# Start of an attention and two-MLP kernel on TensorE: a group of scores placed earlier, two loads issued later, and seven identity products in the gaps

## The reference, cut to what matters

```python
for c in range(nc):                       # chunks of 32 queries
    k_full = np.concatenate([mem_k, k_ctx], axis=2)       # 8 + 16 + 32 + 8 keys
    scores = scale * np.matmul(q_c, k_full.transpose(0, 1, 3, 2))
    a = np.exp(scores - max); a = a / (np.sum(a) + 1e-09)
    out[:, :, c_start:c_end] = np.matmul(a, v_full)
...
h = np.maximum(np.maximum(x @ w1, x @ w2), x @ w3)        # 3072 x 512 x 768, three times
x2 = h @ w_out                                            # 3072 x 768 x 512
h = x2 @ w_in                                             # 3072 x 512 x 2048
g = np.where(h >= 1, h, np.where(h <= -1, 0.0, (h + 1) ** 2 / 4))
return g @ w_out2                                         # 3072 x 2048 x 512
```

## Time and profile before

| what | us |
|---|---|
| median of 3 runs | 960.1 |
| lowest and highest run | 959.87, 960.55 |
| the execution that was profiled | 960.76 |
| its span, first to last instruction | 959.0 |
| TensorE busy in the span | 944.0 |
| GpSimd, DVE, ACT busy | 455.7, 484.2, 434.9 |

### The profile page before, as it was taken

The page is one execution under the profiler, slowest core; times in us unless marked ns, Lnnn a source line. Parts: engine busy times, 40 slices in busy tenths (PEclk is TensorE's granted clock), DMA queues, the critical chain, the costliest instruction groups (busy, mean ns, idle before and its releaser), DMA issues.

```text
span 959.0 us, 19061 instructions
## 1 busy us (share of the span) xinstructions
PE 944.0 (98%) x7806; PEld 877.6 (92%) x7806; DVE 484.2 (50%) x755; ACT 434.9 (45%) x713; POOL 455.7 (48%) x628
## 2 busy tenths in 40 slices
PE   5999999999999999999999999999999999999998
PEld 5999999999999999999989899898999898989897
DVE  4673566667766695761344432545334453423232
ACT  3342343443433443432545555645556463645354
POOL 1668997868986593130232423333332323232321
PEclk9999999999999999999999999999999999999999
DMA  9777899999699778882536445445464443555321
GB/s 373 260 265 245 319 325 387 403 413 397 227 393 383 269 263 304 278 308 103 185 119 226 154 176 187 176 153 184 155 233 144 153 162 137 199 178 182 121 99 66
DMA packets 50327, 223.01 MB, mean 233 GB/s; under 512 B 5952, under 2 KB 10048, under 8 KB 42688
## 3 DMA queue, kind: packets, MB, share of 16 engines
q0 software_dynamic: 31936, 165.17, 48.1%
q1 hardware_dynamic: 18304, 56.63, 16.2%
HBM read 178.00 MB, written 43.78 MB: 231 GB/s over the span
## 4 chain that ended last, share of the span: by engine, by line
PE 95%; DMA 2%; POOL 2%; issue 1%; DVE 0%; ACT 0%; SPq 0%; POOLq 0%
PE mlp_ps L647 21%; PE mlp_ps L648 21%; PE mlp_ps L649 21%; PE attn_ps L649 4%; PE attn_ps L648 4%; PE attn_ps L647 3%; PE scores_ps L649 3%; PE scores_ps L648 3%; PE scores_ps L647 3%; PE attn_ps L640 3%; PE trans_ps L649 2%; PE trans_ps L648 2%; PE trans_ps L647 2%; PE scores_ps L611 2%; DMA wb<-wb_scratch 1%; PE trans_ps L620 1%
## 5 line engine op out<-in xcount | busy, mean ns | idle before, releaser
L936 ACT ACTIVATE up_m<-mlp_ps 128x384 f32<-128x384 f32 x292 | 142.3, 489 | 303.4 <-PE mlp_ps L649 275.0
L647 PE MATMUL mlp_ps<-yc,wa 128*128 128x384 f32 x472 | 160.2, 339 | 0.2 <-issue 0.2
L648 PE MATMUL mlp_ps<-yc,wa 128*128 128x384 f32 x472 | 158.5, 336 | 0.0
L649 PE MATMUL mlp_ps<-yc,wa 128*128 128x384 f32 x472 | 158.0, 335 | 0.0
L544 POOL CAST wo<-wo_raw 128x1024 fp32r<-128x1024 f32 x32 | 33.3, 1039 | 193.5 <-PE trans_ps L649 187.3
L523 POOL DMA_DIRECT2D wa<-wa_scratch x59 | 31.7, 538 | 192.5 <-PE mlp_ps L649 192.4
L647 PE MATMUL mlp_ps<-yc,wb 128*128 128x384 f32 x354 | 119.3, 337 | 0.4 <-DMA wb<-wb_scratch 0.4
L648 PE MATMUL mlp_ps<-yc,wb 128*128 128x384 f32 x354 | 118.9, 336 | 0.0
L649 PE MATMUL mlp_ps<-yc,wb 128*128 128x384 f32 x354 | 118.4, 334 | 0.0
L1537 DVE SCALAR_TENSOR_TENSOR ramp<-ramp,up_m 128x768 f32<-128x768 f32 x62 | 59.5, 959 | 109.1 <-ACT ramp L1187 109.1
L647 PEld LDWEIGHTS mlp_ps<-yc,wa 128*128 128x128 f32 x472 | 88.6, 188 | 7.0 <-ACT up_m L936 0.7
(11 more groups left out here) (178 smaller groups left out, 2178.7 us busy)
## 6 DMA issues: line engine op xcount, KB each, us to landing
wa<-wa_scratch POOLq DMA_DIRECT2D x59, 1024.0 KB, 5.3
wb<-wb_scratch POOLq DMA_DIRECT2D x59, 768.0 KB, 6.8
qk_raw<-qk_l SPq DMA_DIRECT2D x24, 768.0 KB, 8.5
wo_raw<-w_out POOLq DMA_DIRECT2D x32, 512.0 KB, 4.0
wa_scratch<-stage_a POOLq DMA_DIRECT2D x30, 512.0 KB, 5.0
v_raw<-v_l SPq DMA_DIRECT2D x24, 512.0 KB, 7.5
wb_scratch<-stage_a POOLq DMA_DIRECT2D x30, 384.0 KB, 6.9
y_raw<-y_scratch SPq DMA_DIRECT2D x8, 768.0 KB, 5.0
```

Source lines behind the costliest of these rows:

```text
L647: pe.matmul(out_ap, a_hi, b_hi, start=first, stop=False, skip_group_check=beside)
L648: pe.matmul(out_ap, a_lo, b_hi, start=False, stop=False, skip_group_check=beside)
L649: return pe.matmul(out_ap, a_hi, b_lo, start=False, stop=last, skip_group_check=beside)
L936: return act.activation(o, i, ACT.Copy)
```

## The change

There are three edits. First, on TensorE `scores` of group 3 goes from behind the first large product to ahead of it. Second, on SyncE the loads of weight piece 2 and of v of group 3 trade places, and a wait on `attn_done` 2 is put ahead of both. Third, a helper `keep_busy` issues products of the identity with itself (float32, 128x128) into PSUM that nothing reads before it is overwritten: one each behind the scores of groups 0 and 1, two behind those of group 2, one behind the first transposes (with a wait on `sub_done` 2, for the bank), and two behind the transposes of group 1.

```diff
@@ SyncE @@
             load_qk(3)
+            sp.wait_ge(attn_done, 2)
+            load_wa(2)
             load_v(3)
-            load_wa(2)
             load_wa(3)
@@ TensorE, first_tile @@
                     if f == 0:
                         scores_ready(n0, 0, 1)
+                        scores(n0, 0)
                     if r == 0 and j:
                         weighted_v(n0 + j - 1, j - 1)
                         scores(n0 + j, j)
                     layer1(0, 0, f, 0)
-                    if f == 0:
-                        scores(n0, 0)
@@ TensorE, prologue @@
+            def keep_busy(count, bank):
+
+                for _ in range(count):
+                    pe.matmul(bank[:, 0:P], ident[:, :], ident[:, :], start=True, stop=True)
+
             scores_ready(0, 0, 0)
             scores(0, 0)
+            keep_busy(1, trans_ps)
             scores_ready(1, 1, 0)
             scores(1, 1)
+            keep_busy(1, trans_ps)
             scores_ready(2, 2, 0)
             scores(2, 2)
+            keep_busy(2, trans_ps)
             transposes(0, 0)
+            pe.wait_ge(sub_done, 2)
+            keep_busy(1, mlp[0])
             weights_ready(0, 0, 0)
             pe.wait_ge(sub_done, GPT)
             weighted_v(0, 0)
             transposes(1, 1)
+            keep_busy(2, mlp[0])
             transposes(2, 0)
```

## The result

The changed kernel takes 978.1 us (median of six runs, 971.4 to 983.8), the kernel before 960.3 in the same comparison (six runs, 959.9 to 961.7). The ratio on record is 1.0174, with a 95% interval of 1.0152 to 1.0196: 1.7% slower (the quotient of the two medians is 1.0185). The execution that was profiled took 983.76 us with a span of 982.0 us; against the profiled execution of before it lost 23.0 us. It is the slowest of the six, so the trace shows more loss than the 17.8 us between the medians. The forecast was 959.1 us.

A forecast was written before the change was run, and what follows sets the result against it. TensorE was taken as the bound, so time won in the first 28 us passes to the end. The profiled 960.76 us less 1.66 us, the clock gain net of 0.68 us delay, gave 959.1 us; range 956.0 to 960.6.

The forecast's parts named there:

- The scores ahead of the large product: Scores of group 3, moved into TensorE's 0.90 us wait for `x_hi`, run from 21.15 to 22.26 us and cost nothing.
- The loads: SyncE's loads held back by 4.5 us, v of group 3 among them, were needed late; costed at nothing.
- Rival 3: Held loads make GpSimd late, so `wa` lands beyond its 4.7 us of slack; 962.8 us, slower; chance 0.06.
- The clock term: TensorE's clock rises at 25.7 us, with 8 of the first 14 large matmuls slow; net gain 1.66 us.
- The identity products: Seven float32 products in TensorE's prologue, 0.39 us each; those in waits cost nothing, two between transposes cost 0.68 us.
- The 0.68 us of delay at the transposes: Two products between transposes of groups 1 and 2 find no gap and move all behind by 0.68 us (0.42 to 0.94).
- Rival 1: Identity products raise TensorE's clock already in the prologue, so small products run faster; 955.3 to 957.9 us; chance 0.32.
- They cost nothing, even at 0.52: Products behind scores of groups 0 to 2 and the first transposes fit TensorE's waits of 0.6 to 1.4 us.

The follow-up runs named there:

- The first experiment: Kernel before plus seven tiny 32x1 identity products (28 TensorE instructions) ahead of the first scores; 974.7 us, ratio 1.013.
- the run with the whole shift: Changed kernel plus 57 tiny 32x1 identity products ahead of the first scores, shifting the stream by 256 instructions in all; 960.4 us, ratio to before 0.9996.

## Why the prediction was wrong, by its own steps

- **The scores ahead of the large product: right.** In the run with the scores alone they start at 21.27 us and the large product follows at 22.38, with no wait for `x_hi`; forecast were 21.15 and 22.43.
- **The loads: right.** They cost nothing, alone or with the scores. Rival 3 did not happen: `wa` has no wait of its own in the changed kernel. But its slack of 4.7 us was read at the wrong place. GpSimd also loads `wb`, and for that TensorE waits 0.39 us in the kernel before and 0.3 to 1.1 us in six other kernels. So part of a gain made ahead of 198 us can be lost there, as in the run with the scores alone.
- **The clock term: near in size without the identity products, its reason not shown.** The forecast was a rise at 25.7 us and 1.66 us of gain; with scores and loads the rise came at 26.7 and the gain was 0.20% (0.11 to 0.30), 1.9 us. The rise lies anywhere from 26.3 to 28.25 us in kernels whose large product keeps its place and its gap, so that the middle value came near was in part luck. The forecast of 959.1 us was in effect the time of this kernel (958.4).
- **The identity products: near in size, wrong in cost.** At the slow clock the four matmul records of two products take 1.22 us with the pipeline's tail, 0.6 us a product at most (forecast 0.39, at most 0.52), and they lie in the gaps. The 0.68 us of delay at the transposes did not come, since the clock was up and DVE's probabilities were late there.
- **Rival 1 happened as a mechanism.** The clock rose at 11.2 us, weighted v took 1.14 us. The rise came ahead of the first transposes (11.61 us), so these runs do not tell whether transposes count for it. But its sum passed on the gain to the large product. The faster TensorE came to the ends of two pieces, at 18.3 and 22.4 us, before they were there (1.51 and 3.77 us), and the clock was at half from 21.5 to 31.7 us. The scores of group 4 came 2.6 us later than before instead of 4 to 5 us earlier.
- **The step that failed** is "They cost nothing, even at 0.52", with the sentence on which it rests: whatever the first 28 us lose or win is passed on to the end, unless another engine becomes late. In the kernel before, 9.9 of the 15.0 us without work lie ahead of 22.5 us, 3.7 behind TensorE's last matmul and 1.3 between: hardly anything could be won later, but much could be lost. I priced the identity products by their time on TensorE and let the rest of the program stand as it was. What I did not price is that they are instructions: 28 of them move the end of every later piece. The first experiment puts 14 us (974.7 - 960.7) on this alone, and the run with the whole shift, with all edits of the change in it, is back at the time of before (960.4). No rival named it; the chance of 0.06 for slower stood for another mechanism.
- **What of the profile could have told it.** The page of before had the line of 61 packets for the instructions, 16 KB each, and 15,800 records of TensorE over 61 is 259. The timeline had the stall of 0.36 us on "issue" at 103.65, in the middle of a large product, with nothing that it could have waited for. Both were small, but they stood at the edge of a wait that a shift can lengthen to 4.5 us.

**Open.** The six runs of the changed kernel scatter over 12 us where the kernel before scatters over 2. That goes with stalls whose length hangs on how long a packet waits, but I have one trace of each kernel and did not measure it. Why the packet of 300 us began 10 us late was not settled either; with the seven tiny products in front it began 10.6 us late, with the identity products alone 3.7.

## What to carry to other kernels

Where many small products stand close together on TensorE, count its instructions: a float32 product here is four, a transpose two, and an end of 256 that falls behind a piece used up in under some 5 us can cost 0.3 to 5 us, at times with the clock on top. So an instruction added early is costed by what it shifts as well as by its own time, and a change that adds some is tried again with filler up to the next multiple of 256, placed where TensorE waits anyway, before it is thrown away. An idle time on "issue" in the middle of a run of equal matmuls is the sign to look for.

## What the hardware showed that I had not expected

- A stall can cost more than itself. The clock fell 1.7 us behind the first stall of the prologue (1.51 us), just ahead of the second (3.77 us), and was at half until 31.7 us. With those of 2.25, 1.85 and 4.51 us it was at half for 3.4, 3.4 and 6.8 us; behind those of 2.33 us (190 us) and 1.63 us (217 us) it did not fall. The length alone does not decide: with the identity products alone it fell at a stall of 2.06 us and not at one of 2.66.
- Seven identity products in the first 18 us brought the clock up at 9.9 to 11.2 us. Three of them, one wider, did not (25.4 us); nor did the 57 small products (15.5 and 16.3 us) bring it up as early as the seven alone.
- The cost of a tiny product differs with its operands: 57 products with 32 columns of weights from `ident` took 6.2 us, 57 with one column from `half_col` 3.0 us.
